# Network 2's second product, taken by tokens: high and low products side by side, and four turns over the banks instead of eight

## What is computed

```python
x = attn_out.reshape(B * S, D)                 # 8192 x 192
g = x @ w_gate; val = x @ w_val                # network 1, up
x = (g / (1 + exp(-g)) * val) @ w_out          # network 1, down
h = x @ w_in                                   # network 2, up: 192 -> 2048
g = where(h > 0, h, exp(minimum(h, 0)) - 1)
out = g @ w_out                                # network 2, down: 2048 -> 192
```

## Time and profile before

| what | value |
|---|---|
| median of 3 runs | 1221.19 us (1218.65 to 1221.71) |
| the profiled execution | 1220.92 us, of which the span from first to last instruction is 1218.9 us |
| TensorE matmuls | 1213.0 us busy, 11798 instructions |
| weight loads (PEld) | 1079.9 us busy (89%) |
| VectorE, ScalarE, GpSimd | 65%, 55% and 58% busy |
| chain that ended last | TensorE 99% of the span |

### The profile page before, as it was taken

How to read it: one execution, slowest core, us unless ns; L and a number is a source line. 1 busy time by engine, 2 the same in 40 slices (tenths; PEclk the granted TensorE clock), 3 DMA queues, 4 the chain that set the end, 5 groups by cost and what they waited for, 6 DMA issues and landing times.

```text
span 1218.9 us, 31852 instructions
## 1 busy us (share of the span) xinstructions
PE 1213.0 (100%) x11798; PEld 1079.9 (89%) x11798; DVE 787.7 (65%) x1178; ACT 666.9 (55%) x1114; POOL 710.2 (58%) x528
## 2 busy tenths in 40 slices
PE   9999999999999999999999999999999999999999
PEld 7988888889988888899998899999988999998888
DVE  7788565675656766566665666657667575675665
ACT  6557555464554645546465554655546555465554
POOL 7788565474654746547464474654646456465564
PEclk9999999999999999999999999999999999999999
DMA  7412011121101211012110021100212002120110
GB/s 179 116 41 44 19 29 30 31 43 30 26 18 30 43 30 28 15 30 43 30 34 17 22 43 30 37 15 22 43 30 43 9 22 43 30 43 9 31 32 15
DMA packets 103955, 43.37 MB, mean 36 GB/s; under 512 B 75888, under 2 KB 93936, under 8 KB 103920
## 3 DMA queue, kind: packets, MB, share of 16 engines
q1 hardware_dynamic: 103104, 42.29, 15.6%
q10 hardware_dynamic: 816, 0.59, 0.2%
HBM read 16.12 MB, written 6.29 MB: 18 GB/s over the span
## 4 chain that ended last, share of the span: by engine, by line
PE 99%; DVE 1%; ACT 0%; issue 0%; ACTq 0%; DVEq 0%
PE up L860 55%; PE down L860 44%; DVE mixed L830 0%; ACT L617 0%; PE down L1068 0%; DVE mixed L827 0%; DVE taps_head L813 0%; ACTq L615 0%; DVE stage L720 0%; ACT stage L654 0%; ACT taps_exp L617 0%; DVE taps_inv L812 0%; DVE taps_sum L810 0%; DVE taps_eps L811 0%; DVEq L826 0%
## 5 line engine op out<-in xcount | busy, mean ns | idle before, releaser
L441 POOL TENSOR_TENSOR hid_lo<-hidden,hid_hi 128x512 fp32r<-128x512 f32 x447 | 615.4, 1388 | 495.9 <-ACT hid_hi L574 310.8
L734 DVE TENSOR_TENSOR hidden<-act,up 128x512 f32<-128x512 f32 x191 | 130.9, 686 | 248.8 <-ACT act L557 227.1
L771 DVE TENSOR_SCALAR act<-up 128x512 f32<-128x512 f32 x256 | 164.8, 686 | 120.8 <-PE up L860 120.8
L860 PE MATMUL up<-in_b_hi,up_w_hi 64*128 64x512 f32 x1128 | 235.4, 395 | 0.0
L860 PE MATMUL up<-in_b_lo,up_w_hi 64*128 64x512 f32 x1128 | 233.9, 391 | 0.0
L860 PE MATMUL up<-in_b_hi,up_w_lo 64*128 64x512 f32 x1128 | 233.8, 391 | 0.0
L574 ACT ACTIVATE hid_hi<-hidden 128x512 fp32r<-128x512 f32 x192 | 121.6, 633 | 177.4 <-DVE hidden L734 160.2
L608 ACT ACTIVATE hid_hi<-hidden 128x512 fp32r<-128x512 f32 x256 | 158.1, 630 | 104.0 <-DVE hidden L787 82.3
L593 ACT ACTIVATE act<-act 128x512 f32<-128x512 f32 x256 | 157.3, 633 | 95.9 <-DVE act L771 95.9
L860 PE MATMUL down<-out_w,hid_hi 64*128 64x384 f32 x2040 | 204.0, 336 | 0.0
L557 ACT ACTIVATE act<-up 128x512 f32<-128x512 f32 x191 | 114.0, 597 | 157.8 <-PE up L860 155.8
(11 more groups left out here) (96 smaller groups left out, 1155.2 us busy)
## 6 DMA issues: line engine op xcount, KB each, us to landing
x_raw<-x_dram SPq DMA_DIRECT2D x136, 64.0 KB, 2.2
out_dram<-stage SPq DMA_DIRECT2D x15, 384.0 KB, 2.7
in_b_hi<-in_b_hi SPq DMA_DIRECT2D x32, 128.0 KB, 2.3
in_b_lo<-in_b_lo SPq DMA_DIRECT2D x32, 128.0 KB, 2.3
swapped<-halves SPq DMA_DIRECT2D x32, 128.0 KB, 2.2
in_a_hi<-in_a_hi SPq DMA_DIRECT2D x30, 128.0 KB, 2.3
in_a_lo<-in_a_lo SPq DMA_DIRECT2D x30, 128.0 KB, 2.3
stage<-w_out_dram SPq DMA_DIRECT2D x7, 384.0 KB, 4.2
```

The lines of the kernel that those rows point to most:

```text
L441: return pool.tensor_tensor(hid_lo[:, slot, :], hidden[:, s, :], hid_hi[:, slot, :].bitcast(F32), ALU.subtract)
L734: v.tensor_tensor(hidden[:, f % 2, :], act[:, f % 2, :], val_bank(f, n)[:, :], ALU.mult)\
L771: v.tensor_scalar(act[:, k % 2, :], elu_bank(k)[:, :], 0.0, None, ALU.min)\
L860: return nc.tensor.matmul(dst, lhsT, rhs, start=start, stop=stop, skip_group_check=True)
```

## The change

Two things in `down2_pair`, and the same idea in `last_blocks`. First, where one round of four turns made all wide products of the two blocks and a second round all narrow ones, there is now one round in which each turn makes wide k0, narrow k0, wide k0 + 1, narrow k0 + 1. The number and kind of matmuls is unchanged. Second, a stage has four turns instead of eight and two waits on `z_turn` instead of four. Between the turn that is waited for and the turn that waits there lies still one turn, but it is now four couples long (two wide, two narrow) instead of two. Since a stage now ends in the turn (3, 1), every second stage takes its turns in the reverse order, so that it starts where the last one ended.

```diff
             def down2_pair(m, k0):
                 two = (k0, k0 + 1)
-                turns = 4 * (N2 // 2 * m + k0 // 2)
+                turns = 2 * (N2 // 2 * m + k0 // 2)
...
-                for turn, (b, b_low) in enumerate(((0, 2), (1, 3), (2, 0), (3, 1))):
+                order = ((0, 2), (1, 3), (2, 0), (3, 1))
+                for turn, (b, b_low) in enumerate(order if k0 // 2 % 2 == 0 else order[::-1]):
                     if turn >= 2:
                         pe.wait_ge(z_turn, turns + turn - 1)
                     for k in two:
                         pe.wait_ge(hi2_done, N2 * m + k + 1)
-                        end = by_tokens(k, hid_hi, b, b_low, first=k == 0)
-                    if turn < 2:
-                        end.then_inc(z_turn, 1)
-                for turn, (b, b_low) in enumerate(((3, 1), (2, 0), (1, 3), (0, 2))):
-                    if turn >= 2:
-                        pe.wait_ge(z_turn, turns + turn + 1)
-                    for k in two:
+                        by_tokens(k, hid_hi, b, b_low, first=k == 0)
                         pe.wait_ge(lo2_done, N2 * m + k + 1)
                         end = by_tokens(k, hid_lo, b, b_low, last=k == N2 - 1)
                     if turn < 2:
@@
                 down2_pair(CHUNKS - 1, N2 - 4)
                 for b in (0, 1):
-                    for k in two:
-                        whole(b, k, hid_hi)
+                    whole(b, N2 - 2, hid_hi)
                     whole(b, N2 - 2, hid_lo)
+                    whole(b, N2 - 1, hid_hi)
                 for b in (0, 1):
                     whole(b, N2 - 1, hid_lo, True).then_inc(last_z, 1)
                 for b in (2, 3):
                     for k in two:
                         whole(b, k, hid_hi)
-                    whole(b, N2 - 2, hid_lo)
-                    whole(b, N2 - 1, hid_lo, True).then_inc(last_z, 1)
+                        last = whole(b, k, hid_lo, k == N2 - 1)
+                    last.then_inc(last_z, 1)
```

## The result

The changed kernel took 1206.78 us (1206.01 to 1207.07, 4 runs) against 1221.45 us for the one before; the ratio is 0.9883, 95% interval 0.9866 to 0.99. That is 14.7 us or 1.2% faster. I had said 1210.4 us, 10.8 us faster, with a range of 1204 to 1216.

What follows compares the result with a forecast made beforehand. TensorE, busy 1213.0 of 1218.9 us, was taken to bound the kernel; the stall gone and alternation neutral gave 127 x 0.085 = 10.8 us off 1220.9, plus 0.3 for the median: 1210.4 us, range 1204 to 1216 for 8 in 10.

Steps and rivals of the forecast that it cites:

- step 1: Narrow round's `z_turn` wait on TensorE: its stall of 0.09 us goes in every stage, 127 x 0.09 = 11.4 us.
- step 2: Alternating wide and narrow couples in a stage: 0.29 us for both kinds either way, so alternation gives nothing.
- Rival A: Weight load hidden when kinds alternate in a stage: 0.263 us for both, 35 us gained, 1186 us; chance 0.08.
- rival C: Both prices paid in a stage: 0.32 us for both kinds, 19 us slower, 1240 us; chance 0.05.
- The isolated matmul gap: Skill's rule for TensorE, N / 2.4 + 2.5 ns: a stage of 1.96 us in any order, against 2.38 traced.
- The sum: Whole kernel: 0.085 us gained a stage, 127 x 0.085 = 10.8 us, giving 1210.4 us, 0.9% less.
- The seven stages: Stages whose lower rows run about 0.15 us behind: 0.09 us still left before the `z_turn` wait would stall.
- step 3: Narrow loads in a stage want GpSimd's low parts earlier; least margin 0.49 us, so cost nothing.
- `last_blocks`, sequencer instructions: Last blocks' six moved matmuls: nothing within 0.05 us; fewer waits and register instructions on TensorE's sequencer: nothing.

Runs made afterwards that it cites:

- Experiment 3: Kernel before the change, its narrow round's turns reordered so the third takes over the bank of the turn right before it; 1248.02 us, ratio 1.0232.
- experiment 2: Changed kernel with eight turns of two couples and four `z_turn` waits a stage, wide and narrow still alternating; 1212.37 us, ratio 0.9936.
- experiment 1: Changed kernel, but inside a turn both wide couples come first, then both narrow ones; 1205.89 us, ratio 0.9886.
- experiment 4: Changed kernel with narrow couples of 128 columns instead of 192 in `down2_pair`; 1209.02 us, ratio 0.9908.
- experiment 5: Changed kernel with narrow couples of 256 columns instead of 192; 1213.79 us, ratio 0.996.
- experiment 8: Changed kernel with the last two blocks of the last chunk (`last_blocks`) in the old order; 1206.42 us, ratio 0.9904.
- experiment 7: Changed kernel, wide couples first within a turn, one chunk 1 low part made by GpSimd instead of VectorE, the next a step later; 1207.51 us, ratio 0.9909.

## Why the prediction was right, and where it was off

*The stall on `z_turn`* (step 1): right in place and kind. It is gone in every stage; the load starts 0.57 us behind the awaited couple in the changed kernel (0.58 was forecast), where 0.31 to 0.34 would do. Experiment 3 enlarges it, experiment 2 brings a small one back, experiment 1 shows that removing it is enough.

*The alternation* (step 2): right. 0.29 for both kinds was taken, 0.287 measured, and experiments 1, 4 and 5 show it from three sides: the order within the turn is neutral, fewer columns bring nothing, more columns are paid only past the load. Rival A (0.263) and rival C (0.32) are both out: the narrow couple's 0.09 and the wide one's 0.20 are one load and one plain wide couple, cut at another place. The Trainium skill, page "TensorE: Matmul & The Clock Gate", section "LDWEIGHTS (loading the stationary operand)", gives a load's time as its columns / 1.2, an estimated 107 ns for 128 columns; the loads here are 0.10 to 0.11 us apart behind a narrow start, so the trace agrees. The isolated matmul gap of the same page, section "Back-to-back issue gap", which I had set against my rows, has no load in it, as that section says itself; its estimate for both kinds was 0.245 us, 0.287 was measured, and experiment 4 shows that the load is what decides.

*The sum*: here a size was off. "I take 0.085 us" a stage was 0.106 us, so 13.5 us instead of 10.8. I had added seven times 0.29 from rows of two decimals, and 0.287 alone makes 0.02 us a stage of it. So the stall's 0.08 is most of the gain, and the rest is spread over the couples in hundredths that such rows don't resolve. That the total still lay in the range has some luck in it: 1.0 us from the seven longer stages and 1.9 from outside the stages were not forecast, and the 1.2 lost in chunk 1 and the later start of 1.36 us took most of them back.

*The seven stages* with late lower rows: the prediction took the lag of 0.15 us as one that stays, and put no time to it. In the changed kernel no stage of network 2 has it.

*The early demand for the low parts* (step 3): "cost nothing" held in the profiled executions of experiments 1, 2 and 8 and failed in that of the changed kernel, at the very stage that I had named as the one of least slack. I had taken GpSimd's margin of 0.49 us as the only one. But the first 0.63 us are lost by an up block that waits for VectorE, and only the other 0.58 by a narrow couple that waits for GpSimd's low part; both come behind the subtraction that took 3.63 us instead of 2.04, and neither is there in experiment 8. It cost 1.2 us once, and it need not come. What the two engines contend for no run here shows. All later chunks have over 0.7 us of slack at the start of a stage, and TensorE waits for nobody there.

*`last_blocks`, sequencer instructions*: nothing, as expected (experiment 8).

*What the prediction did not have*: 1.9 us outside the stages, below.

## What to carry to other kernels

Read the cost of short matmuls from the distance between starts, and compare it with the distance between weight loads: here a matmul with few moving columns cost its successor's load (0.11 us for 128 stationary columns of 4 bytes), and neither fewer columns nor another order bought anything below that. Where two row halves swap accumulator banks, count the time from the last matmul of the turn that is waited for to the first load of the turn that waits. In these runs the load could start 0.06 us after that matmul's end in the trace, which is 0.31 to 0.33 us after its start with 192 columns and 0.40 with 384. If less lies between, it stalls, and behind short matmuls there is no room that would absorb it, while behind long ones there is. Longer turns cost nothing on TensorE here (experiment 1); so lengthen the turn before looking for finer tricks, and look at which operands are then wanted earlier.

## What the runs showed of the hardware beside this

*A wait inside TensorE's queue has no name in the views while it is short.* The stall of 0.08 us in each of 127 stages shows as no idle time and no wait in the earlier trace rows; only the distance between loads has it. At 0.3 us, in experiment 3, it is named.

*Blocks outside the stages got faster.* In network 1 a block of 28 matmuls took 3.253 us or 3.267 us, with its 14 distances alternately 0.238 and 0.229 in the longer kind and between 0.228 and 0.241 in the shorter. In the kernel before, 56 of 128 such blocks were of the longer kind, all eight of a chunk or none (timeline of TensorE, start of the down part of two such blocks):

```profile
436.22 0.86 PE L860 MATMUL down<-hid_hi,out_w 64*128 64x512 f32 x6
...
439.49 0.86 PE L860 MATMUL down<-hid_hi,out_w 64*128 64x512 f32 x6
```

In the changed kernel it was 2 (two of the usual ones):

```profile
433.75 0.85 PE L860 MATMUL down<-hid_hi,out_w 64*128 64x512 f32 x6
437.00 0.86 PE L860 MATMUL down<-hid_hi,out_w 64*128 64x512 f32 x6
```

In experiment 3, with the larger stall, it was 113 of 128, in experiments 1, 2 and 5 few, in experiment 4 some 40. The instructions of these blocks are the same in all. It goes with stalls in narrow rounds, but experiment 4 has none of them; the cause stays open.

In the kernel before, from chunk 2 on, the seven chunks without longer blocks are just those in which the lower rows fall behind the upper ones, by 0.013 us a block, and whose first stage takes 2.52 us. So a chunk of before lost 0.11 to 0.15 us in one way or the other, and one of the changed kernel in neither. The longer blocks are 54 x 0.0135 = 0.7 us of the 1.9 from outside the stages. Another 0.7 are 13 up blocks, one in a chunk, that took 2.17 us before and 2.12 now; the rest is spread over network 1. Rows that run apart need not cost anything: in most of experiment 8 the two matmuls of a couple start 0.09 to 0.11 us apart, and a stage with its up block takes 4.387 us there as in the changed kernel.

*The start differs by 1.3 us between executions of the same instructions.* Eight transposes at the start took 1.09 us in the kernel before and 1.97 in the changed one (timeline of TensorE, first before, then changed, whose line numbers are five lower):

```profile
4.90 1.09 PE L1068 MATMUL down<-ident,stage 128*128 128x128 f32 x8
```

```profile
5.30 1.97 PE L1063 MATMUL down<-ident,stage 128*128 128x128 f32 x8
```

The view of the clock gives 1.00 for both stretches, but the trace's own records of the granted clock begin only at 4.10 us in the kernel before and at 9.49 us in the changed one, both with 1.00; the view takes a stretch without a record for full speed. The starts say what was granted there. The twelve matmuls of 128 columns from 1.26 us on start 0.213 us apart in both executions; the transposes, of the same form, start 0.109 us apart in the kernel before and 0.213 in the changed one, about twice as long, which is the step between the 2.4 and the 1.2 GHz level. So the changed kernel's start ran at the low level for some 5 us longer, and the "full clock in every stretch" of the section on the chip does not hold for this one. TensorE had done the same matmuls before in both, so the difference is no property of the change.

Experiments 3 and 7, with records from 4.92 and 4.49 us on, were of the short kind, the others, from 9.17 to 10.63 us on, of the long one. Only the profiled executions have a trace; whether this start and the loss in chunk 1 make the spread between runs of one kernel is not shown.
